# Second scores, transposes and weighted sums change places in the feature block of a fused attention and two-MLP kernel

## The reference, cut to what matters

```python
# 4 batches x 8 heads, 768 tokens, head size 64; 8 memory keys and values
for c in range(24):                       # chunks of 32 queries
    k_full = concat(mem_k, k[c_start-16 : c_end+8])      # at most 64 keys
    scores = q_c @ k_full.T / sqrt(64)
    a = softmax(scores)                   # max subtracted, sum + 1e-9
    out_c = a @ v_full
x = tokens x 512                          # 3072 tokens
h = max(x @ w1, x @ w2, x @ w3)           # 512 -> 768
y = h @ w_out1                            # 768 -> 512
u = y @ w_in2                             # 512 -> 2048
g = u if u >= 1; 0 if u <= -1; else (u + 1)**2 / 4
out = g @ w_out2                          # 2048 -> 512
```

## Time and profile before

| | |
|---|---|
| median of 3 runs | 1145.23 us (1142.74 to 1145.8) |
| span of the profiled execution | 1141.5 us |
| median less that span | 3.7 us |
| TensorE busy | 1065.2 us (93%) |
| VectorE busy | 614.5 us (54%) |
| ScalarE busy | 453.1 us (40%) |
| GpSimd busy | 181.3 us (16%) |

### The profile page before, as it was taken

How to read it: one execution, slowest core, us unless ns; L and a number is a source line. 1 busy time by engine, 2 the same in 40 slices (tenths; PEclk the granted TensorE clock), 3 DMA queues, 4 the chain that set the end, 5 groups by cost and what they waited for, 6 DMA issues and landing times.

```text
span 1141.5 us, 17089 instructions
## 1 busy us (share of the span) xinstructions
PE 1065.2 (93%) x6072; PEld 985.5 (86%) x6072; DVE 614.5 (54%) x1374; ACT 453.1 (40%) x915; POOL 181.3 (16%) x100
## 2 busy tenths in 40 slices
PE   3588998989989898999999999999999999999998
PEld 2478987889888898899999999999999999999997
DVE  5858476584866848567145434344444434444343
ACT  5645354353543534444433333333333323233322
POOL 4452122121221212120355000000000000000000
PEclk9679999999999999999999999999999999999999
DMA  9823222242222422320344000100000010000000
GB/s 253 236 73 104 87 79 70 82 118 80 71 85 66 121 88 61 93 74 2 120 146 141 28 28 1 56 0 28 28 28 28 0 55 0 28 28 1 28 0 28
DMA packets 27327, 75.28 MB, mean 66 GB/s; under 512 B 3712, under 2 KB 7808, under 8 KB 27264
## 3 DMA queue, kind: packets, MB, share of 16 engines
q1 hardware_dynamic: 27264, 74.46, 21.8%
HBM read 61.87 MB, written 12.58 MB: 65 GB/s over the span
## 4 chain that ended last, share of the span: by engine, by line
PE 78%; DVE 11%; ACT 5%; issue 3%; DMA 2%; SPq 0%; ACTq 0%; DVEq 0%
PE mlp L458 16%; PE mlp L460 16%; PE mlp L459 16%; PE scores_ps L460 5%; PE scores_ps L459 5%; PE scores_ps L458 5%; DVE row_den L870 5%; PE attn_ps L451 4%; PE trans_ps L459 3%; PE trans_ps L460 3%; PE trans_ps L458 3%; ACT x_f L592 2%; PE scores_ps L417 2%; PE trans_ps L440 2%; DVE prob L874 1%
## 5 line engine op out<-in xcount | busy, mean ns | idle before, releaser
L458 PE MATMUL mlp<-x_hi,w_hi 128*128 128x384 f32 x576 | 201.6, 350 | 1.1 <-DVE x_lo L880 1.1
L460 PE MATMUL mlp<-x_lo,w_hi 128*128 128x384 f32 x576 | 195.2, 339 | 0.0
L459 PE MATMUL mlp<-x_hi,w_lo 128*128 128x384 f32 x576 | 194.8, 338 | 0.0
L779 ACT ACTIVATE squared<-clamped,half_col 128x384 f32<-128x384 f32 x128 | 79.0, 617 | 255.5 <-DVE clamped L974 255.5
L460 PE MATMUL mlp<-y_lo,w_in_hi 128*128 128x384 f32 x512 | 172.5, 337 | 0.0
L458 PE MATMUL mlp<-y_hi,w_in_hi 128*128 128x384 f32 x512 | 172.2, 336 | 0.0
L459 PE MATMUL mlp<-y_hi,w_in_lo 128*128 128x384 f32 x512 | 171.8, 336 | 0.0
L974 DVE TENSOR_SCALAR clamped<-mlp 128x384 f32<-128x384 f32 x128 | 71.2, 556 | 133.3 <-PE mlp L460 133.3
L976 DVE TENSOR_TENSOR g_f<-squared,mlp 128x384 f32<-128x384 f32 x128 | 70.9, 554 | 87.6 <-ACT squared L779 87.6
L978 DVE TENSOR_TENSOR g_lo<-g_f,g_hi 128x384 fp32r<-128x384 f32 x128 | 72.5, 567 | 81.6 <-ACT g_hi L592 81.6
L458 PEld LDWEIGHTS mlp<-x_hi,w_hi 128*128 128x128 f32 x576 | 109.3, 190 | 3.9 <-issue 1.5
(11 more groups left out here) (81 smaller groups left out, 1689.6 us busy)
## 6 DMA issues: line engine op xcount, KB each, us to landing
k_raw<-k_l SPq DMA_DIRECT2D x48, 320.0 KB, 4.8
q_raw<-q_l SPq DMA_DIRECT2D x48, 256.0 KB, 4.0
v_raw<-v_l SPq DMA_DIRECT2D x24, 512.0 KB, 3.4
y_scratch<-y_stage SPq DMA_DIRECT2D x32, 192.0 KB, 1.9
y_raw<-y_scratch SPq DMA_DIRECT2D x8, 768.0 KB, 4.3
out<-out_stage SPq DMA_DIRECT2D x24, 256.0 KB, 2.1
stage_a<-w SPq DMA_DIRECT2D x12, 384.0 KB, 6.4
stage_b<-w_in SPq DMA_DIRECT2D x16, 256.0 KB, 2.9
```

The lines of the kernel that those rows point to most:

```text
L458: pe.matmul(out_ap, a_hi, b_hi, start=first, stop=False)
L459: pe.matmul(out_ap, a_lo, b_hi, start=False, stop=False)
L460: return pe.matmul(out_ap, a_hi, b_lo, start=False, stop=last)
L779: act.activation(squared[:, f % 2], clamped[:, f % 2], ACT.Square, bias=half_col[:, 0:1], scale=0.5).then_inc(square_done, 1)
```

## The change

On TensorE, the second scores of a block now always follow its first matmul block (before: in block 0 only; in the others after the second). The transposes of the unit before follow the second matmul block (before: the first), and its weighted sums follow the third (before: they stood ahead of it). On ScalarE the second raw copy stands ahead of `h_first`, and `x_out` at the end of the block, behind the split and the exponent. On VectorE the second pack stands ahead of `h_second` in all blocks, and `x_low` behind `softmax_scale`. No instruction is added or removed.

```diff
@@ TensorE, tile_a @@
                     layer1(t, a, f, 0)
-                    if attention and f:
-                        transposes(n0 + f - 1, (f - 1) % 2)
-                    if attention and f == 0:
+                    if attention:
                         scores_halves(n0 + f, f % 2, 1, g0 + f // UPG, slot_of(f))
                     layer1(t, a, f, 1)
                     if attention and f:
-                        scores_halves(n0 + f, f % 2, 1, g0 + f // UPG, slot_of(f))
+                        transposes(n0 + f - 1, (f - 1) % 2)
+                    layer1(t, a, f, 2)
                     if attention and f:
                         attend(f - 1)
-                    layer1(t, a, f, 2)
                 layer2(t, a, 0)
@@ ScalarE, tile_a @@
                     if f:
                         h_high(t, f - 1)
+                    raw_copy(n0 + f, 1)
                     h_first(t, a, f)
                     if f:
                         transposed(n0 + f - 1)
-                    raw_copy(n0 + f, 1)
-                    if f:
-                        x_out(n0 + f - 1, (f - 1) % 2, 1 - a, (f - 1) // UPG)
                     if j < (k_splits if r else q_splits):
                         split_ahead(g0 + j, r, (a + 1 + j) % 2)
                     exponent(n0 + f, f % 2)
+                    if f:
+                        x_out(n0 + f - 1, (f - 1) % 2, 1 - a, (f - 1) // UPG)
@@ VectorE, tile_a @@
                         h_low(t, f - 1)
-                    if f:
-                        h_second(t, a, f)
                     if attention:
                         pack_half(n0 + f, 1, tg)
-                    if not f:
-                        h_second(t, a, f)
+                    h_second(t, a, f)
                     if attention:
                         softmax_shift(n0 + f, True)
-                        if f:
-                            x_low(n0 + f - 1, (f - 1) % 2, (f - 1) % 2, 1 - a, (f - 1) // UPG)
                     if f == KF1 - 1:
                         h_third(t, a, f)
                         h_low(t, f)
                     if attention:
                         softmax_scale(n0 + f, f % 2)
+                        if f:
+                            x_low(n0 + f - 1, (f - 1) % 2, (f - 1) % 2, 1 - a, (f - 1) // UPG)
```

## The result

| | before | after |
|---|---|---|
| median, us | 1144.15 (4 runs, 1142.74 to 1145.8) | 1180.07 (4 runs, 1176.72 to 1182.14) |
| span of the profiled execution, us | 1141.5 | 1179.8 |

The ratio is 1.0309, with a 95% interval of 1.0287 to 1.0331: 36 us slower, where 19 were forecast and 1172 us was the upper end of the range.

A forecast was written before the change was run, and what follows sets the result against it. It took TensorE's 38.4 us of waits for probabilities, with VectorE held until GpSimd finishes, as the bound. Six loop tiles adding 14.2 us and the last attention tile 4.9 made 19.1, hence 1164 us; range 1154 to 1172.

The forecast's parts named there:

- What bounds the kernel: TensorE's transposes wait 38.4 us for probabilities in split blocks, because VectorE is held until GpSimd finishes the split.
- T: Moment when a block's second scores have been issued on TensorE; T to T is one block's step.
- terms (2) to (4): Blocks with a split: second scores wait for a pack delayed by later GpSimd; k 10.65 us against 10.09, q 9.97 against 9.40.
- term (5): Blocks without a split: x_low decides when the pack ends; step 9.33 us against 8.39, plus 0.94.
- terms (6) and (7): A tile's first step changes by minus 0.84 us; its last transposes by plus 0.97, plus 2.75 in the last attention tile.
- the terms for that last tile: Last attention tile's end: ScalarE's h copy behind x_out, then VectorE's wait and low part, ending about T + 7.95.
- the bound for x_low: Uncertainty from x_low taking 0.33 or 0.42 us on VectorE: 0.04 in each of 35 steps, plus or minus 1.5 us.
- the third rival: TensorE idling up to 2.3 us lowers its clock: up to 5 us per tile, 35 in seven, 1199 us; chance 0.06.
- SP's queue is not touched: Claim that SP's DMA queue is unchanged and its loads wait for the same counts; no cost was assigned.

The follow-up runs named there:

- e5: Kernel before the change, with ScalarE's exponent moved ahead of the split: 1116.71 us, ratio 0.9761.
- e4: Changed kernel with ScalarE's split moved ahead of the transposed copies, so that GpSimd starts earlier: 1162.17 us, ratio 1.0149.
- e10: e3 with x_low on VectorE moved behind the next block's first pack and h_low: 1156.4 us, ratio 1.0101.
- e3: Changed kernel with both the filler matmuls of e1 and the later load of v of e2: 1165.74 us, ratio 1.0188.
- e1: Changed kernel with seven unread matmuls ahead of the second scores in every block but a tile's first: 1171.01 us, ratio 1.0223.
- e2: Changed kernel with each load of v issued one group later, behind the next load of k on SP: 1175.86 us, ratio 1.0287.
- e9: e4 together with the later load of v of e2: 1149.43 us, ratio 1.0037.
- e7: Changed kernel with exponent ahead of the split, x_out and x_low one block later, and the later load of v of e2: 1109.48 us, ratio 0.9699.

## Why the prediction was wrong, point by point

1. *What bounds the kernel* was right. Taking away what it named, VectorE held until GpSimd's end, took every probability wait out of the blocks and 27 us off the kernel before (e5).
2. *The step from T to T*, terms (2) to (4): 10.65 and 9.97 forecast, 10.64 and 9.93 measured. e4 moves GpSimd's start and the step follows; e10 moves x_low and the step loses its 0.33.
3. *Without a split*, term (5): 9.33 forecast, 9.62 measured. x_low decides, as forecast:

```profile
568.46 0.43 DVE L878 TENSOR_TENSOR x_lo<-x_f,x_hi 128x256 fp32r<-128x256 f32 x1 [1.53 <-ACT x_hi L590]
...
568.80 0.55 DVE L889 TENSOR_TENSOR h_max<-h_max,mlp 128x384 f32<-128x384 f32 x1
...
569.41 0.09 DVE L841 MEMSET score<- 32x32 f32 x1
```

VectorE waits 1.53 us for x_hi. The 0.29 are the weighted sums 0.12 later than I took them (T + 4.62) and, behind h_third, a memset that only groups at the edge of a batch have and that now lies in front of the pack. The same memset adds 0.2 to two steps in each even tile.
4. *The first step and the end of a tile*, terms (6) and (7): 8.53 against 8.43, and the last transposes at T + 9.37 (193.66 to 203.03) against 9.22. In the last attention tile they came at T + 9.29 against 9.20. Small, but they come in nearly every tile. Two slips of the working are smaller still: the terms for that last tile add up to 7.99, not 7.95, and the bound for x_low counts 35 steps where 28 have it.
5. Points 3 and 4 make 0.7 (first steps), 1.0 (tile ends), 0.6 (no split) and 1.3 (memsets): 3.6 us, and 19.1 + 3.6 is close to the 22.6 by which e3's span, 1164.1, stands above that of before.
6. *The clock*, the third rival, is the step that failed. I argued that waits of 1.5 us had never lowered the granted clock and that TensorE stays over three quarters busy. It did fall, eight times in tiles 1 to 6, behind some of the gaps of 1.97 to 2.22 us and those of 2.73 and 2.94 where k was late. The page could not have shown such stretches: 3 us at half clock take 0.05 off a slice of 29 us, which stays a 9, and of the eight only the two that share the ninth slice show there. (The trace of the kernel before does have 1.00 from 130 to 620 us.) I had also made it one case among exclusive ones, with 0.06 and a price of 35 us, when it adds to the forecast: it came to 9 us here (e1), 1.1 to 1.6 for each stretch.
7. *SP's queue is not touched*, in the first paragraph on the change, was the other failed step. The program of SP is unchanged, but its load of v waits for a count that the moved weighted sums give, and the load of k is queued behind it. Alone that is 0.5 to 0.9 us in three steps; with the longer gaps and the clock behind them it was 4 to 5 us by the medians (e2, and e3 against e1), whose single runs overlap. e9 against e4 shows 13 us for it where the split comes early.
8. Points 6 and 7 together are 14.3 us (e3), and they are what put the time outside the range. With the 21.6 that e3 keeps they give the 35.9.

What remains open is why the clock fell behind one gap of 1.97 us and not behind another of 1.99. The runs show only that in tiles 1 to 6 it did not happen where the gaps were filled down to 1.39 us or less (e3) or gone (e7).

## What to carry to other kernels

Before moving a step on the engine that is the bound, follow the loop that closes through the other engines: here the new order only exchanged one wait for another, and put two more operations (x_low, and the wait for the transposed copies) into the same loop. The cheap lever was elsewhere, an exchange of two operations on ScalarE that let the short operations on VectorE pass before GpSimd began. And when a step moves, look for every wait on its semaphore, in the queues of loads too, and for what stands behind that wait. A wait on the bound engine that grows can cost clock on top of its own length: that is a term to add, not a case beside the others.

## What the runs showed of the hardware that was not expected

- TensorE at full clock and 88% busy (60.66 of 69 us, from 91 to 160) dropped to half clock for some 3 us behind a gap of 1.97 us (0.85 over that block). It did so behind three of six waits of 1.69 to 1.77 us in e5, and not behind one of 1.99 us in the changed kernel. With 0.9 us of otherwise useless matmuls in each gap the clock stayed up in all but two places, and the kernel was 9 us faster (e1).
- GpSimd's split held three kinds of operation of VectorE with two inputs in SBUF, the subtraction 1.56 us, x_low 1.60 and h_low 0.95, and also row_den, 2.23 us, which reads only the four row sums and a constant. Each ended 0.02 to 0.42 us after GpSimd. Others passed: the row sum just ahead of row_den, one input in SBUF, took its 0.42 us while GpSimd was at work, and in e5 a maximum (L891, 0.56 us) and a pack (1.10), each with one input in PSUM, ran at their usual length. Why row_den is held and the row sum is not, the runs do not show.
